# The second projection in two runs of 18 matmuls per quad, and the gate's column sums made by TensorE

## The chip, the cores and the metric

The kernel runs on one core of a Trainium2 chip. The metric is the device time of one execution, in microseconds (us). Five engines work from queues of their own, each in the order in which the program gives it its instructions: TensorE (PE in the profile, its weight loads PEld), VectorE (DVE), ScalarE (ACT), GpSimd (POOL) and SyncE (SP), which only issues transfers here. They wait for each other by semaphores.

## What is computed

Three stages in float32 on 1536 tokens of 512 features: attention in chunks with a few memory rows, then two mixtures of experts that use every expert. The second mixture's gate is normalized eight times in turn over the experts of a token and over all the tokens of an expert.

```python
# mixture 1: E = 4 experts, F = 1024 hidden features
p = domain_probs / (domain_probs.sum(-1, keepdims=True) + 1e-09)
for e in range(E):
    h = np.maximum(x @ w1[e], 0.0)
    out += p[:, e:e + 1] * (h @ w2[e])
...
# mixture 2: E = 8 experts
logits = x @ w_gate
logits = logits - logits.max()
P = np.exp(logits)
for _ in range(8):
    P /= P.sum(1, keepdims=True) + 1e-09
    P /= P.sum(0, keepdims=True) + 1e-09
    P *= N / E
for e in range(E):
    h = np.maximum(x @ w1[e], 0.0)
    out += P[:, e:e + 1] * (h @ w2[e])
```

## The kernel before

**Precision.** Every large product is made of three matmuls on rounded values: an operand is split into hi (a rounded copy, made by ScalarE) and lo (the value less hi, made by VectorE), and `in_three` adds hi x lo, hi x hi and lo x hi.

**Order of the mixtures.** There are four passes (mixture 1 for batch 0 and 1, mixture 2 for batch 0 and 1), of 4, 4, 8 and 8 experts. An expert is four quads, so there are 96 quads, numbered 0 to 95: passes begin at quads 0, 16, 32 and 64. A quad is a 2 x 2 block of the first projection (256 hidden features, 768 tokens), done in seven products instead of eight by Strassen's scheme. Each product is 6 matmuls of 384 columns into the PSUM areas c_ps[0] to c_ps[3]. Two quads fill one buffer h of hidden values, 512 features, called half m.

**The work on a quad.** GpSimd forms four sums of weight blocks (`sum_s`), ScalarE splits the seven stationary blocks (`split_s`, s_hi, L610) and VectorE makes the lo part (s_lo, L749). TensorE runs products 0 to 6. ScalarE copies four partial results out of PSUM (`keep_part`, L628), VectorE adds each to another area (`add`, L768), ScalarE applies the relu and rounds (`hidden`, h_hi, L632), and VectorE makes h_lo (L772). The four (add, hidden) pairs belong to products 2, 5, 6 and 7, counted from one, so the last needs the quad's last product. The first product of the next quad needs its s_lo, and the PSUM areas of the first two pairs.

**The second projection** (`down`) of half m runs during the quads 2m+2 and 2m+3: in each of them three tiles of 128 tokens, each of 4 x 3 matmuls of 512 columns into one of three areas y_ps. It is cut into pieces of three matmuls, and `PIECES` says how many stand behind each product. VectorE adds each finished tile to the result (`accumulate`, L784 to L790). It needs w2 split in the same way (`split_w2`, by ScalarE in L615 and VectorE in L755).

```python
PIECES = (2, 2, 1, 2, 2, 2, 1)
...
                    product(quad, i)
                    for _ in range(PIECES[i]):
                        if m >= 0:
                            down(m, piece // 4, piece % 4)
                        piece += 1
```

**Between passes.** The tokens of the next pass are summed (`sum_t`, `sum_t4` on GpSimd) and split (`split_t`, L623 and L760) in the last quad of a pass (15, 31, 63), each block when the product that last used its buffer is done (`next_tokens`). Behind mixture 1 TensorE transposes the rows (`turn_rows`) and makes the logits, in quads 18 and 33 to 34.

**The gate.** The largest logit over all tokens is found on GpSimd at quad 34 (L368). The eight rounds are cut into nine slots, three in each of quads 35, 36 and 37 (`gates`): VectorE normalizes over experts and sums a token column (`sinkhorn_rows`, L805 to L809), GpSimd sums over the 128 partitions (L372), and VectorE takes the sum up (`sinkhorn_columns`, L813 to L817). GpSimd's wait for a column sum stands in the same queue as `sum_s`.

**The queues.** All orders are written out by hand. w1_raw and w2_raw are single buffers: SP loads w1 of quad q when s_lo of quad q-1 is made, and w2 of half m when the last w2_lo of half m-1 is made.

Of the kernel before, what the change touches and what calls it, by code (L numbers as in the profile page):

```python
# [11 lines left out]
RED = bass.bass_isa.ReduceOp  # L12
# [25 lines left out]
PIECES = (2, 2, 1, 2, 2, 2, 1)  # L38


def build(nc, q, k, v, mem_k, mem_v, domain_probs, a_w1, a_w2, w_gate, b_w1, b_w2, out):
# [37 lines left out]
    with ExitStack() as ctx:  # L79
# [29 lines left out]
        ident = sb("ident", [P, P])  # L109
        gate = sb("gate", [P, TILES, E])  # L110
# [3 lines left out]
        cols = sb("cols", [P, 3 * EB])  # L114
# [24 lines left out]
        csum, ctotal, crec = cols[:, 0:EB], cols[:, EB:2 * EB], cols[:, 2 * EB:3 * EB]  # L139
# [36 lines left out]
        lmax_ready, gmax_ready, nmax_ready, sink_exp = sem("lmax_ready"), sem("gmax_ready"), sem("nmax_ready"), sem("sink_exp")  # L176
        csum_ready, ctotal_ready = sem("csum_ready"), sem("ctotal_ready")
# [5 lines left out]
        for t in range(ST):  # L183
            TURNS[LAST_A[0] + 2, t] = ("turn", 0, t)
        TURNS[LAST_A[0] + 2, 6] = ("logits", 0, 0)
        for t, (dq, i) in enumerate(((1, 0), (1, 1), (1, 2), (1, 4), (2, 0), (2, 1))):
            TURNS[LAST_A[1] + dq, i] = ("turn", 1, t)
        TURNS[LAST_A[1] + 2, 3] = ("logits", 1, 0)
        SINK0 = LAST_A[1] + 3

# [101 lines left out]
        def _(pool):  # L292
# [3 lines left out]
                               pattern=[[-1, P]], channel_multiplier=1).then_inc(ident_ready, 1)  # L296
            pool.memset(k_in[1][:], 0.0).then_inc(k_in_zeroed[1], 1)
# [59 lines left out]
            sum_s(1)  # L357
            for quad in range(ALLQ):
                for p in range(1, PASSES):
                    if quad == QUADS * (FIRST[p] - 1):  # L360
                        sum_t(p)
                    if quad == QUADS * FIRST[p] - 1:
                        sum_t4(p)
                if quad + 2 < ALLQ:
                    sum_s(quad + 2)
                if quad == SINK0 - 1:
                    pool.wait_ge(lmax_ready, 1)
                    pool.partition_all_reduce(gmax, lmax, P, RED.max).then_inc(gmax_ready, 1)  # L368
                if SINK0 <= quad < SINK0 + 3:
                    for it in range(3 * (quad - SINK0), min(3 * (quad - SINK0) + 3, SINKHORN)):  # L370
                        pool.wait_ge(csum_ready, it + 1)
                        pool.partition_all_reduce(ctotal, csum, P, RED.add).then_inc(ctotal_ready, 1)  # L372

        @block.tensor
        def _(pe):
# [91 lines left out]
            def down(m, t, f):  # L467

                y, par = m * ST + t, m % 2
                if t == 0 and f == 0:  # L470
                    pe.wait_ge(h_lo_ready, 8 * (m + 1))
                    pe.wait_ge(w2_lo_ready, 2 * (m + 1))
                if f == 0 and y >= 3:
                    pe.wait_ge(y_taken, y - 2)
                ts = slice(t * P, (t + 1) * P)
                mm = in_three(y_ps[y % 3], h_hi[par][:, f, ts], h_lo[par][:, f, ts], w2_hi[par][:, f, :],
                              w2_lo[par][:, f, :], f == 0, f == 3)
                if f == 3:
                    mm.then_inc(y_summed, 1)

# [47 lines left out]
            for quad in range(ALLQ):  # L528
                m = quad // 2 - 1
                piece = 12 * (quad % 2)  # L530
# [39 lines left out]
        def _(act):  # L570
# [102 lines left out]
            for quad in range(ALLQ):  # L673
                take_turned(quad, 0)
# [4 lines left out]
                take_turned(quad, 1)  # L679
                next_tokens(quad, 1)  # L680
                hidden(quad, 0)
                take_turned(quad, 2)
                keep_part(quad, 1)
                next_tokens(quad, 2)
                take_turned(quad, 3)
                split_w2(quad // 2, quad % 2)
                keep_part(quad, 2)
                next_tokens(quad, 3)
                take_turned(quad, 4)
                keep_part(quad, 3)  # L690
                next_tokens(quad, 4)
                hidden(quad, 1)
                take_turned(quad, 5)
                hidden(quad, 2)
                next_tokens(quad, 5)
                hidden(quad, 3)
                next_tokens(quad, 6)
                if quad == SINK0 - 1:
                    act.wait_ge(nmax_ready, 1)
                    act.activation(sink[:], sink[:], ACT.Exp, bias=nmax).then_inc(sink_exp, 1)  # L700

        @block.vector
        def _(dve):
# [47 lines left out]

            def split_w2(m, j):
                dve.wait_ge(w2_hi_ready, 2 * m + j + 1)
                fs = slice(2 * j, 2 * j + 2)
                dve.tensor_tensor(out=w2_lo[m % 2][:, fs, :], in0=w2_raw[:, fs, :], in1=w2_hi[m % 2][:, fs, :].bitcast(F32),  # L755
                                  op=ALU.subtract).then_inc(w2_lo_ready, 1)
# [54 lines left out]
            def sinkhorn_columns(it):  # L811
                dve.wait_ge(ctotal_ready, it + 1)
                then(dve.tensor_scalar(crec, ctotal, EPS, None, ALU.add))  # L813
                then(dve.reciprocal(crec, crec))
                then(dve.tensor_scalar(crec, crec, N / EB, None, ALU.mult))
# [52 lines left out]
            for quad in range(ALLQ):  # L868
                m, t0 = quad // 2 - 1, 3 * (quad % 2)
                if m >= 1 or quad == 3:  # L870
                    accumulate((quad - 1) // 2 - 1, 3 * ((quad - 1) % 2) + 2)
                if quad == SINK0 + 3:
# [17 lines left out]
                if (quad, 3) in TURNS and TURNS[quad, 3][0] == "logits":  # L890
                    take_logits(TURNS[quad, 3][1])
                gates(quad, 1)
                add(quad, 1)
                hidden(quad, 1)
                if m >= 0:
                    accumulate(m, t0 + 1)
                next_tokens(quad, 4)
                add(quad, 2)
                hidden(quad, 2)
                next_tokens(quad, 5)  # L900
                add(quad, 3)
                hidden(quad, 3)
                next_tokens(quad, 6)
                if (quad, 6) in TURNS:
                    take_logits(TURNS[quad, 6][1])
                if quad == SINK0 - 1:
                    dve.wait_ge(gmax_ready, 1)
                    dve.tensor_scalar(nmax, gmax, -1.0, None, ALU.mult).then_inc(nmax_ready, 1)
                gates(quad, 2)
# [24 lines left out]
```

## Time and profile before

| | |
|---|---|
| median of 3 runs | 1722.59 us (1720.34 to 1725.53) |
| the profiled execution | 1730.89 us |
| its span | 1729.1 us |
| mean granted TensorE clock | 0.963 |
| PE busy | 1626.9 us (94%) |
| DVE busy | 1003.6 us (58%) |
| ACT busy | 690.9 us (40%) |
| POOL busy | 329.8 us (19%) |

The span runs from the first to the last instruction of the program, and the profiled execution's time has 1.8 us around it. Windows and timelines count from the span's start. Matmuls overlap in the profile (one of 384 columns is shown as 0.33 long, and the next starts 0.17 to 0.18 behind it), so starts are to be compared, not lengths. A granted clock (PEclk) of 1.00 is 2.4 GHz, and 0.50 is 1.2 GHz.

### The profile page before, as it was taken

What the parts mean: (1) busy time and instruction counts of PE and PEld (TensorE: products, weight loads), DVE (VectorE), ACT (ScalarE), POOL (GpSimd) and SP (SyncE); (2) the same over time, 40 slices, a digit from 0 to 9 for tenths busy, and PEclk for the clock granted to TensorE, in tenths of its full rate; (3) what the DMA queues carried; (4) which work ended last, traced back from release to release, by engine and by line L of the source; (5) the groups of instructions that cost most, each with busy time, mean ns of one, the idle gap of its engine ahead of it and who ended that gap; (6) DMA issues with size and microseconds to landing.
All of it is one profiled execution on the core that took longest, in us unless ns stands there. A gap on an engine that the chain in (4) does not pass through costs nothing.

```text
span 1729.1 us, 21400 instructions
## 1 busy us (share of the span) xinstructions
PE 1626.9 (94%) x8673; PEld 1448.9 (84%) x8673; DVE 1003.6 (58%) x1445; ACT 690.9 (40%) x1058; POOL 329.8 (19%) x429
## 2 busy tenths in 40 slices
PE   6659999989999989759999999998999999999999
PEld 6648888879888879648888888887888888888887
DVE  5455655664565564536656565657565556556563
ACT  5443344443334443213444434434334443444441
POOL 2211113121111322011111111132111111111110
PEclk9779999999999999889999999999999999999999
DMA  9832122211212221111121222121222121121210
GB/s 161 127 67 85 62 62 72 62 49 49 86 61 62 73 61 49 40 46 49 61 73 62 61 86 62 49 85 49 97 85 61 50 86 61 56 79 62 78 57 37
DMA packets 158930, 117.75 MB, mean 68 GB/s; under 512 B 31336, under 2 KB 129640, under 8 KB 158832
## 3 DMA queue, kind: packets, MB, share of 16 engines
q1 hardware_dynamic: 158832, 116.39, 23.9%
q8 instruction: 68, 1.11, 0.3%
q14 instruction: 30, 0.25, 0.1%
HBM read 113.22 MB, written 3.15 MB: 67 GB/s over the span
## 4 chain that ended last, share of the span: by engine, by line
PE 85%; DVE 5%; SPq 3%; issue 2%; DMA 2%; ACT 1%; POOL 1%; POOLq 0%
PE banks L439 28%; PE banks L441 28%; PE banks L440 28%; SPq L229 1%; DVE t_lo L760 1%; DVE s_lo L749 1%; SPq L228 1%; DMA w_raw<-in_moe_w 1%; PE banks L497 1%; DVE banks L768 1%; ACT h_hi L632 1%; DMA v_bd<-in_mem_v 1%; DVE h_lo L772 1%; PE banks L425 0%; PE banks L489 0%
## 5 line engine op out<-in xcount | busy, mean ns | idle before, releaser
L439 PE MATMUL banks<-t_lo,s_hi 128*128 128x384 f32 x1344 | 459.6, 342 | 35.9 <-DVE h_lo L772 33.3
L439 PE MATMUL banks<-w_lo,h_hi 128*128 128x512 f32 x1152 | 459.7, 399 | 20.6 <-DVE h_lo L772 19.9
L440 PE MATMUL banks<-w_hi,h_hi 128*128 128x512 f32 x1152 | 459.5, 399 | 0.0
L441 PE MATMUL banks<-w_hi,h_lo 128*128 128x512 f32 x1152 | 458.7, 398 | 0.0
L441 PE MATMUL banks<-t_hi,s_lo 128*128 128x384 f32 x1344 | 456.9, 340 | 0.0
L440 PE MATMUL banks<-t_hi,s_hi 128*128 128x384 f32 x1344 | 454.5, 338 | 0.0
L768 DVE TENSOR_TENSOR banks<-banks,part 128x384 f32<-128x384 f32 x384 | 216.3, 563 | 362.7 <-PE banks L441 220.9
L632 ACT ACTIVATE h_hi<-banks 128x384 fp32r<-128x384 f32 x384 | 188.9, 492 | 555.3 <-DVE banks L768 555.3
L628 ACT ACTIVATE part<-banks 128x384 f32<-128x384 f32 x384 | 188.8, 492 | 392.8 <-PE banks L441 392.6
L439 PEld LDWEIGHTS banks<-t_lo,s_hi 128*128 128x128 f32 x1344 | 256.5, 191 | 67.1 <-issue 36.4
L772 DVE SCALAR_TENSOR_TENSOR h_lo<-banks,h_hi 128x384 fp32r<-128x384 f32 x384 | 213.4, 556 | 163.7 <-ACT h_hi L632 163.7
L307 POOL TENSOR_TENSOR w_raw<-w_raw 128x256 f32<-128x256 f32 x96 | 72.3, 753 | 1206.0 <-DMA w_raw<-in_moe_w 1206.0
L440 PEld LDWEIGHTS banks<-t_hi,s_hi 128*128 128x128 f32 x1344 | 256.1, 191 | 28.0
L439 PEld LDWEIGHTS banks<-w_lo,h_hi 128*128 128x128 f32 x1152 | 219.0, 190 | 59.3 <-DVE h_lo L772 35.8
L441 PEld LDWEIGHTS banks<-w_hi,h_lo 128*128 128x128 f32 x1152 | 218.5, 190 | 48.8
L441 PEld LDWEIGHTS banks<-t_hi,s_lo 128*128 128x128 f32 x1344 | 255.8, 190 | 0.0
L790 DVE SCALAR_TENSOR_TENSOR rows<-banks,gate,rows 128x512 f32<-128x512 f32 x258 | 192.3, 745 | 82.1 <-PE banks L441 82.1
L440 PEld LDWEIGHTS banks<-w_hi,h_hi 128*128 128x128 f32 x1152 | 218.8, 190 | 23.2
L749 DVE TENSOR_TENSOR s_lo<-w_raw,s_hi 128x1792 fp32r<-128x1792 f32 x96 | 193.5, 2016 | 0.0
L610 ACT ACTIVATE s_hi<-w_raw 128x1792 fp32r<-128x1792 f32 x96 | 162.6, 1694 | 2.1 <-POOL w_raw L312 2.1
L755 DVE TENSOR_TENSOR w_lo<-w_raw,w_hi 128x1024 fp32r<-128x1024 f32 x96 | 117.0, 1219 | 2.4 <-ACT w_hi L615 2.4
L615 ACT ACTIVATE w_hi<-w_raw 128x1024 fp32r<-128x1024 f32 x96 | 101.0, 1052 | 0.0
(87 smaller groups left out, 642.5 us busy)
## 6 DMA issues: line engine op xcount, KB each, us to landing
w_raw<-in_moe_w SPq DMA_DIRECT2D x192, 256.0 KB, 3.2
w_raw<-in_moe_w SPq DMA_DIRECT2D x48, 1024.0 KB, 7.0
v_bd<-in_v SPq DMA_DIRECT2D x16, 308.0 KB
w_raw<-in_q SPq DMA_DIRECT2D x8, 384.0 KB, 6.0
k_in<-in_k SPq DMA_DIRECT2D x8, 384.0 KB
out_x<-rows SPq DMA_DIRECT2D x12, 256.0 KB, 2.8
v_bd<-in_mem_v SPq DMA_DIRECT2D x16, 48.0 KB
v_bd<-in_v SPq DMA_DIRECT2D x16, 10.0 KB
```

The source lines that it names most:

```text
L439: pe.matmul(out_, lhs_hi, rhs_lo, start=start, stop=False, skip_group_check=chained)
L440: pe.matmul(out_, lhs_hi, rhs_hi, start=False, stop=False, skip_group_check=chained)
L441: return pe.matmul(out_, lhs_lo, rhs_hi, start=False, stop=stop, skip_group_check=chained)
L610: act.activation(s_hi[quad % 2][:], w1_raw[:, 1:PRODUCTS + 1, :, :], ACT.Copy).then_inc(s_hi_ready, 1)
L615: act.activation(w2_hi[m % 2][:, 2 * j:2 * j + 2, :], w2_raw[:, 2 * j:2 * j + 2, :], ACT.Copy).then_inc(w2_hi_ready, 1)
L628: act.activation(part[:, j, :], c_ps[(0, 0, 3, 0)[j]], ACT.Copy).then_inc(part_copied, 1)
L632: act.activation(hidden_at(h_hi, quad, k), c_ps[BLOCKS[k][0]], ACT.Relu).then_inc(h_hi_ready, 1)
L749: dve.tensor_tensor(out=s_lo[quad % 2][:], in0=w1_raw[:, 1:PRODUCTS + 1, :, :], in1=s_hi[quad % 2][:].bitcast(F32), op=ALU.subtract).then_ ...
L755: dve.tensor_tensor(out=w2_lo[m % 2][:, fs, :], in0=w2_raw[:, fs, :], in1=w2_hi[m % 2][:, fs, :].bitcast(F32), op=ALU.subtract).then_inc(w ...
L768: dve.tensor_tensor(out=bank, in0=bank, in1=part[:, (0, 2, 3, 1)[k], :], op=ALU.add).then_inc(c_added, 1)
L772: dve.scalar_tensor_tensor(out=hidden_at(h_lo, quad, k), in0=c_ps[BLOCKS[k][0]], scalar=0.0, in1=hidden_at(h_hi, quad, k).bitcast(F32), op ...
L790: dve.scalar_tensor_tensor(out=dst, in0=got, scalar=by, in1=dst, op0=ALU.mult, op1=ALU.add).then_inc(y_taken, 1)
```

## The change

- The second projection of a quad is no longer spread over all seven products. Its three tiles stand in two runs of 18 matmuls, one behind the fourth product (i == 3) and one behind the seventh.
- ScalarE and VectorE make the split of the next quad's stationary blocks (`split_s`) behind the quad's last `hidden`, where it stood near the quad's beginning. ScalarE's part of `split_w2` follows it, and so do the token splits 2 to 6 of a pass's last quad.
- The lo part of w2 (`split_w2`) moves from VectorE to GpSimd. SP's order of loads is unchanged, and a w2 load now waits for GpSimd's part.
- The gate's sums over the partitions are made by TensorE: a matmul of a matrix of ones with the columns' sums, into PSUM (`column_sums`), read there by VectorE. Two scalings of the reciprocal are folded into one instruction. The sums stand behind the first run, behind the seventh product, and behind the sixth matmul of the second run.
- The largest logit is found with a transpose, a VectorE reduction and a matmul that spreads it (`turn_largest`, `spread_largest`).
- The transposes and logits move by one product, the rescaling of quad 38 moves behind `hidden(quad, 0)`, and `accumulate` moves with the runs.

```diff
-PIECES = (2, 2, 1, 2, 2, 2, 1)
+TILES_BEHIND = 3
...
-        TURNS[LAST_A[0] + 2, 6] = ("logits", 0, 0)
...
+            TURNS[LAST_A[0] + 2, t + 1] = ("turn", 0, t)
+        TURNS[LAST_A[0] + 3, 1] = ("logits", 0, 0)
+        for t in range(ST):
+            TURNS[LAST_A[1] + 1 + t // 3, t % 3 + 1] = ("turn", 1, t)
+        TURNS[LAST_A[1] + 2, 4] = ("logits", 1, 0)
...
+        COLUMN_SUMS = {}
+        for it in range(SINKHORN):
+            COLUMN_SUMS[SINK0 + it // 3, (4, 7, 9)[it % 3]] = it
+        RESCALE = SINK0 + 3
...
+            def split_w2(m, j):
+                pool.wait_ge(w2_hi_ready, 2 * m + j + 1)
+                fs = slice(2 * j, 2 * j + 2)
+                pool.tensor_tensor(out=w2_lo[m % 2][:, fs, :], in0=w2_raw[:, fs, :],
+                                   in1=w2_hi[m % 2][:, fs, :].bitcast(F32), op=ALU.subtract).then_inc(w2_lo_ready, 1)
             for quad in range(ALLQ):
+                if quad + 1 < ALLQ:
+                    sum_s(quad + 1)
...
-                if quad + 2 < ALLQ:
-                    sum_s(quad + 2)
-                if quad == SINK0 - 1:
-                    pool.wait_ge(lmax_ready, 1)
-                    pool.partition_all_reduce(gmax, lmax, P, RED.max).then_inc(gmax_ready, 1)
-                if SINK0 <= quad < SINK0 + 3:
-                    for it in range(3 * (quad - SINK0), min(3 * (quad - SINK0) + 3, SINKHORN)):
-                        pool.wait_ge(csum_ready, it + 1)
-                        pool.partition_all_reduce(ctotal, csum, P, RED.add).then_inc(ctotal_ready, 1)
+                split_w2(quad // 2, quad % 2)
...
+            def turn_largest():
+                pe.wait_ge(lmax_ready, 1)
+                pe.transpose(x_ps[0:1, P:2 * P], lmax, ident[:]).then_inc(lmax_turned, 1)
+
+            def spread_largest():
+                pe.wait_ge(gmax_ready, 1)
+                pe.wait_ge(ones_ready, 1)
+                pe.matmul(x_ps[:, 2 * P:2 * P + 1], ones[0:1, :], gmax[0:1, :], start=True, stop=True).then_inc(gmax_spread, 1)
+
+            def column_sums(it):
+
+                pe.wait_ge(csum_ready, it + 1)
+                if it == 0:
+                    pe.wait_ge(ones_ready, 1)
+                pe.matmul(x_ps[:, 0:EB], ones[:], csum, start=True, stop=True).then_inc(ctotal_ready, 1)
...
+                    if (quad, i) in COLUMN_SUMS:
+                        column_sums(COLUMN_SUMS[quad, i])
                     product(quad, i)
-                    for _ in range(PIECES[i]):
-                        if m >= 0:
-                            down(m, piece // 4, piece % 4)
-                        piece += 1
+                    if i == 3 and m >= 0:
+                        down(m, t0, range(4))
+                        down(m, t0 + 1, range(2))
+                if quad == SINK0 - 1:
+                    turn_largest()
+                if (quad, PRODUCTS) in COLUMN_SUMS:
+                    column_sums(COLUMN_SUMS[quad, PRODUCTS])
+                if m >= 0:
+                    down(m, t0 + 1, range(2, 4))
+                if quad == SINK0 - 1:
+                    spread_largest()
+                if (quad, PRODUCTS + 2) in COLUMN_SUMS:
+                    column_sums(COLUMN_SUMS[quad, PRODUCTS + 2])
+                if m >= 0:
+                    down(m, t0 + 2, range(4))
...
                 keep_part(quad, 0)
                 next_tokens(quad, 0)
+                take_turned(quad, 1)
+                next_tokens(quad, 1)
+                take_turned(quad, 2)
+                hidden(quad, 0)
+                keep_part(quad, 1)
+                take_turned(quad, 3)
+                keep_part(quad, 2)
+                take_turned(quad, 4)
+                keep_part(quad, 3)
+                take_turned(quad, 5)
+                hidden(quad, 1)
+                take_turned(quad, 6)
+                hidden(quad, 2)
+                hidden(quad, 3)
                 if quad + 1 < ALLQ:
                     split_s(quad + 1)
...
                 split_w2(quad // 2, quad % 2)
...
+                for i in range(2, PRODUCTS):
+                    next_tokens(quad, i)
...
+                if quad > 2:
+                    accumulate((quad - 1) // 2 - 1, TILES_BEHIND * ((quad - 1) % 2) + 2)
+                gates(quad, 0)
+                next_tokens(quad, 0)
+                add(quad, 0)
+                next_tokens(quad, 1)
+                hidden(quad, 0)
...
+                gates(quad, 1)
                 if m >= 0:
                     accumulate(m, t0)
...
+                add(quad, 1)
+                add(quad, 2)
+                hidden(quad, 1)
+                add(quad, 3)
+                hidden(quad, 2)
+                hidden(quad, 3)
+                gates(quad, 2)
...
                 if quad + 1 < ALLQ:
                     split_s(quad + 1)
                 next_tokens(quad, 2)
...
                 next_tokens(quad, 3)
...
                 if m >= 0:
                     accumulate(m, t0 + 1)
...
+                for i in range(4, PRODUCTS):
+                    next_tokens(quad, i)
```

## Rows read from the trace of the kernel before

**Rows 1.** Busy time by stretch: window and length, engines (instructions), PEclk, DMA share, GB/s

```profile
152.84:1692.33 1539.49, 1491.54 (x7322) 1328.60 (x7321) 911.69 (x1300) 616.31 (x954) 293.42 (x385) 0.98 0.21 64
957.59:973.26 15.67, 15.67 (x79) 14.10 (x78) 9.44 (x14) 6.47 (x10) 2.87 (x4) 1.00 0.33 101
973.26:989.21 15.95, 15.93 (x80) 14.05 (x78) 9.45 (x14) 6.48 (x10) 2.87 (x4) 1.00 0.11 33
358.21:381.50 23.29, 18.57 (x79) 16.26 (x78) 14.37 (x20) 8.31 (x13) 3.61 (x5) 0.85 0.16 53
381.50:439.75 58.25, 58.25 (x308) 53.09 (x306) 28.60 (x41) 22.78 (x36) 8.59 (x12) 0.94 0.20 64
652.39:694.62 42.23, 42.23 (x227) 38.67 (x226) 19.16 (x28) 16.05 (x26) 6.07 (x9) 0.92 0.17 50
694.62:799.51 104.89, 71.86 (x314) 62.64 (x312) 54.89 (x132) 25.58 (x41) 14.73 (x24) 0.82 0.13 41
```

**Rows 2.** Timeline of quads 49 and 50: start, length, engine, line, what, [idle before]

```profile
971.69 0.33 PE L440 MATMUL banks<-t_hi,s_hi 128*128 128x384 f32 x1
...
972.39 0.34 PE L441 MATMUL banks<-t_hi,s_lo 128*128 128x384 f32 x1
...
972.76 0.57 DVE L768 TENSOR_TENSOR banks<-banks,part 128x384 f32<-128x384 f32 x1 [0.35 <-PE banks L441]
...
973.36 0.49 ACT L632 ACTIVATE h_hi<-banks 128x384 fp32r<-128x384 f32 x1 [1.54 <-DVE banks L768]
...
973.88 0.56 DVE L772 SCALAR_TENSOR_TENSOR h_lo<-banks,h_hi 128x384 fp32r<-128x384 f32 x1 [0.56 <-ACT h_hi L632]
...
974.50 0.50 PE L439 MATMUL banks<-w_lo,h_hi 128*128 128x512 f32 x1
974.51 0.49 ACT L628 ACTIVATE part<-banks 128x384 f32<-128x384 f32 x1 [0.66 <-PE banks L441]
...
974.83 0.39 PE L440 MATMUL banks<-w_hi,h_hi 128*128 128x512 f32 x1
...
974.90 1.70 ACT L610 ACTIVATE s_hi<-w_raw 128x1792 fp32r<-128x1792 f32 x1
...
983.84 0.49 ACT L628 ACTIVATE part<-banks 128x384 f32<-128x384 f32 x1 [1.94 <-PE banks L441]
...
984.43 0.57 DVE L768 TENSOR_TENSOR banks<-banks,part 128x384 f32<-128x384 f32 x1 [1.54 <-ACT part L628]
```

**Rows 3.** Timeline of quad 31, then one line of GpSimd's groups by line

```profile
620.84 2.02 DVE L749 TENSOR_TENSOR s_lo<-w_raw,s_hi 128x1792 fp32r<-128x1792 f32 x1
...
621.00 3.56 POOL L339 TENSOR_TENSOR rows<-rows,t_two 128x768 f32<-128x768 f32 x1 [7.95 <-DVE t_lo L760]
...
622.78 2.60 DVE L760 TENSOR_TENSOR t_lo<-t_two,t_hi 128x768 fp32r<-128x768 f32 x1
...
L331 POOL TENSOR_TENSOR rows<-rows 128x768 f32<-128x768 f32 x4 | 7.4, 1842 | 0.0
```

**Rows 4.** Timeline of quad 35's gate slot, then one line of the DMA issues

```profile
715.51 0.42 POOL L372 PARTITION_ALL_REDUCE cols<-cols  x1 [6.01 <-issue]
715.97 0.17 DVE L813 TENSOR_SCALAR cols<-cols 128x8 f32<-128x8 f32 x1 [12.05 <-POOL cols L372]
...
717.95 0.32 DVE L809 TENSOR_REDUCE cols<-sink 128x8 f32<-128x96 f32 x1
...
w_raw<-in_moe_w SPq DMA_DIRECT2D x192, 256.0 KB, 3.2
```

**Rows 5.** TensorE's gaps in the timeline, and the stretches behind them

```profile
32.66 0.44 PE L425 MATMUL banks<-v_bd,p_t 128*32 128x130 f32 x4 [3.79 <-DMA v_bd<-in_mem_v]
...
1709.23 0.50 PE L439 MATMUL banks<-w_lo,h_hi 128*128 128x512 f32 x1 [1.07 <-DVE h_lo L772]
...
32.10:35.40 3.30, 2.74 (x52) 2.77 (x56) 0.00 (x0) 0.00 (x0) 0.70 (x1) 0.50 1.15 101
1708.20:1728.00 19.80, 16.64 (x72) 13.44 (x72) 5.72 (x8) 0.39 (x1) 0.00 (x0) 1.00 0.20 75
```

More of the change, by code:

```diff
@@ L11 @@
 AX = mybir.AxisListType
-RED = bass.bass_isa.ReduceOp
 CHUNK, LEFT, RIGHT = 32, 16, 8
@@ L109, in build @@
         ident = sb("ident", [P, P])
+        ones = sb("ones", [P, P])
         gate = sb("gate", [P, TILES, E])
@@ L138, in build @@
         tok_sum = small[:, 24:36]
-        csum, ctotal, crec = cols[:, 0:EB], cols[:, EB:2 * EB], cols[:, 2 * EB:3 * EB]
+        csum, crec = cols[:, 0:EB], cols[:, EB:2 * EB]
         lmax, gmax, nmax = small[:, 48:49], small[:, 49:50], small[:, 50:51]
@@ L465, in product, with down @@
                 mm.then_inc(prod_done, 1)
-            def down(m, t, f):
+            def down(m, t, fs):
                 y, par = m * ST + t, m % 2
-                if t == 0 and f == 0:
+                if t == 0 and fs[0] == 0:
                     pe.wait_ge(h_lo_ready, 8 * (m + 1))
                     pe.wait_ge(w2_lo_ready, 2 * (m + 1))
-                if f == 0 and y >= 3:
+                if y >= 3 and fs[0] == 0:
                     pe.wait_ge(y_taken, y - 2)
                 ts = slice(t * P, (t + 1) * P)
-                mm = in_three(y_ps[y % 3], h_hi[par][:, f, ts], h_lo[par][:, f, ts], w2_hi[par][:, f, :],
-                              w2_lo[par][:, f, :], f == 0, f == 3)
-                if f == 3:
+                for f in fs:
+                    mm = in_three(y_ps[y % 3], h_hi[par][:, f, ts], h_lo[par][:, f, ts], w2_hi[par][:, f, :],
+                                  w2_lo[par][:, f, :], f == 0, f == 3)
+                if fs[-1] == 3:
                     mm.then_inc(y_summed, 1)
+            def turn_largest():
[10 more added lines that the diff above has]
+                pe.matmul(x_ps[:, 0:EB], ones[:], csum, start=True, stop=True).then_inc(ctotal_ready, 1)
             def turn_rows(b, t):
@@ L528, in _ @@
             for quad in range(ALLQ):
-                m = quad // 2 - 1
-                piece = 12 * (quad % 2)
+                m, t0 = quad // 2 - 1, TILES_BEHIND * (quad % 2)
                 for i in range(PRODUCTS):
@@ L750, in split_s @@
                                   in1=s_hi[quad % 2][:].bitcast(F32), op=ALU.subtract).then_inc(s_lo_ready, 1)
[L752 to L756, printed above, removed]
             def split_t(p, i):
@@ L812, in sinkhorn_columns @@
                 dve.wait_ge(ctotal_ready, it + 1)
-                then(dve.tensor_scalar(crec, ctotal, EPS, None, ALU.add))
+                then(dve.tensor_scalar(crec, x_ps[:, 0:EB], EPS, EB / N, ALU.add, ALU.mult))
                 then(dve.reciprocal(crec, crec))
-                then(dve.tensor_scalar(crec, crec, N / EB, None, ALU.mult))
                 dst = gate[:, :, EA:E] if it == SINKHORN - 1 else sink[:]
@@ L868, in _ @@
             for quad in range(ALLQ):
[L869 to L872, printed above, removed]
+                m, t0 = quad // 2 - 1, TILES_BEHIND * (quad % 2)
+                if quad > 2:
[5 more added lines that the diff above has]
+                hidden(quad, 0)
+                for i in (1, 4):
+                    if TURNS.get((quad, i), ("",))[0] == "logits":
+                        take_logits(TURNS[quad, i][1])
+                if quad == RESCALE:
                     dve.wait_ge(y_taken, (HALVES * FIRST[2] + 2) * ST)
@@ L877, in _ @@
                     dve.wait_ge(rescaled, ST)
-                gates(quad, 0)
-                next_tokens(quad, 0)
-                add(quad, 0)
+                gates(quad, 1)
                 if m >= 0:
                     accumulate(m, t0)
-                hidden(quad, 0)
-                next_tokens(quad, 1)
+                add(quad, 1)
[5 more added lines that the diff above has]
+                gates(quad, 2)
+                if quad == SINK0 - 1:
+                    dve.wait_ge(lmax_turned, 1)
+                    dve.tensor_reduce(gmax[0:1, :], x_ps[0:1, P:2 * P], AX.X, ALU.max).then_inc(gmax_ready, 1)
                 if quad + 1 < ALLQ:
@@ L887, in _ @@
                 next_tokens(quad, 2)
-                split_w2(quad // 2, quad % 2)
+                if quad == SINK0 - 1:
+                    dve.wait_ge(gmax_spread, 1)
+                    dve.tensor_scalar(nmax, x_ps[:, 2 * P:2 * P + 1], -1.0, None, ALU.mult).then_inc(nmax_ready, 1)
                 next_tokens(quad, 3)
[L890 to L894, printed above, removed]
                 if m >= 0:
                     accumulate(m, t0 + 1)
[L897 to L909, printed above, removed]
+                for i in range(4, PRODUCTS):
+                    next_tokens(quad, i)
             accumulate(ALLM - 2, ST - 1)
```

35 lines of the change are left out of this document (6 added, 29 removed).

## The prediction

> **What bounds the kernel now.** I read the stretches first, cut at the starts of quads (a quad begins with the first matmul of its first product). In quad 49 TensorE is busy for all of 15.67 us, and quad 50 takes 15.95 [rows 1]. Every quad holds the same 42 product matmuls and 36 of the second projection, so 15.67 is the floor that the matmuls alone set. From quad 3 to quad 94 the stretch is 1539.5 us, and 92 floors are 1441.6: the excess is 97.9 us [rows 1]. Its parts, from the same view:
> - Quads that carry nothing special and have an even number lose 0.28 (15.95 against 15.67), and there are 39 of them: 10.9.
> - The first quad behind each change of tokens or mixture (16, 32, 64) takes some 23 us (quad 16 stands for the three), 7.3 to 7.6 over the floor: 22.5 for three.
> - Quads 17 to 19 take 58.25 (11.2 over three floors), 33 and 34 take 42.23 (10.9 over two). They carry the transposes and the logits.
> - Quads 35 to 38, the gate's eight rounds, take 104.9: 42.2 over four floors, with TensorE busy for 71.9.
>
> That makes 97.7. The timeline of quads 49 and 50 then shows the 0.28: h_lo of the quad before ends at 974.44, and the second projection's first matmul starts at 974.50 instead of right behind the product; it takes 0.50 where its neighbour takes 0.39, because its weight load too stood behind the wait [rows 2]. So TensorE is the bound, and a change to its order can gain at most what is in the list; what it can lose has no such limit.
>
> **The change, part by part.** *The second projection behind products four and seven.* The floor stays: the same 78 matmuls. A product costs 6 x 0.175 = 1.05 (four product matmuls start from 971.69 to 972.39, in steps of 0.17 to 0.18 [rows 2]); the other 36 matmuls have 15.67 - 7.35 = 8.32, so 0.231 each, and a run of 18 is 4.16. What goes away is the 0.28 of the even quads: the first of these matmuls now stands three products (3.15 us) later, and h_lo was 0.18 late. Gain 10.9.
>
> *split_s behind the last hidden, on ScalarE and on VectorE.* Today ScalarE makes the next quad's s_hi right behind the first part copy (974.51, then 974.90 [rows 2]), some ten microseconds ahead of its use. Now it comes after hidden(3), which waits for the last add, which waits for the seventh product. The next quad's first product waits for s_lo. So there is a chain from the seventh product to the next first product, and it runs beside 18 matmuls. Count from S, the start of the seventh product's last matmul:
> - S to the last add. A free VectorE starts 0.37 later (972.39, 972.76 [rows 2]). Here it isn't free. From the fifth product's last start: its part is copied after 0.37 and the add starts 0.59 behind the copy's start (983.84, 984.43), so at 0.96; h_hi 0.60 later, h_lo 0.52 later still (972.76, 973.36, 973.88), at 2.08; the engine takes its next instruction 0.08 before one ends (620.84 plus 2.02 against 622.78 [rows 3]), so at 2.56. S is at 2.10. I take 0.46; lower bound 0.37.
> - add to h_hi 0.60, and h_hi to s_hi 0.39 as from 974.51 to 974.90 [rows 2].
> - s_hi 1.70 [rows 2], 0.03 to the next engine (h_hi's end at 973.85, h_lo at 973.88), s_lo 2.02 [rows 3], 0.06 to TensorE (974.44 to 974.50).
>
> Sum 5.26. TensorE is free at 0.17 + 4.16 = 4.33. It waits 0.93, and a start from a wait costs 0.10 more (0.50 against 0.39 [rows 2]): **1.03 per quad**, 94.8 for the 92 quads. Bounds: with 0.37 in the first step, 0.94; above, if one more hand-over of 0.2 is in it (part copy and add stand 0.10 further apart than a copy's 0.49), 1.25. Before, nothing hung on this chain, so the trace has no such wait; it's made of its rows.
>
> *split_w2 from VectorE to GpSimd.* GpSimd takes 1.84 for 768 columns alone [rows 3], so 2.46 for 1024. Its input, w2_hi, comes from ScalarE right behind s_hi; by columns against s_hi (1024 to 1792 in 1.70) that is 1.0, so it is ready while s_lo still runs. At 620.84 VectorE's s_lo began first and took its usual 2.02, GpSimd's instruction came 0.16 later and took 3.56, and VectorE's next two-operand one 2.60 [rows 3]: the second of two stands until the first is through. So s_lo isn't slowed, GpSimd starts at its end and is done 2.5 later; the second projection needs w2_lo 4.3 after the same moment (four products). Hidden with 1.8 to spare; without it, a shortfall would cost once in two quads. VectorE loses 1.2 us of work per quad that was on nobody's path.
>
> The Trainium skill, "GPSIMD Engine Reference", section Key points, says that GpSimd shares its SBUF interfaces with VectorE and contends with instructions that have two SBUF inputs. It does not say who gives way; taken as both being slowed while they overlap, it gives the third rival below, and by it the sum would be some 100 us higher than by the row.
>
> *The loads.* SP's next w1 load waits for s_lo as before. It lands 3.2 after issue [rows 4] and GpSimd's four sums of 256 columns need less than 1 each (1.84 for 768 [rows 3]), so s_summed comes at most 7.2 behind s_lo; ScalarE asks for it 16.7 - 3.8 = 13 behind. The w2 load waits for GpSimd now, 2.5 later than s_lo, and stands ahead only of a w1 load that is due a quad later. Nothing.
>
> *Start, quads 0 and 1.* No second projection exists yet, so nothing covers the chain: quad 1 and quad 2 each begin 5.3 behind S, and after idle of that length the clock is low. In quad 16 idle of 4.7 (23.29 less 18.57 busy) came with a mean clock of 0.85 [rows 1], so 7 us at half, and 7.6 - 4.7 = 2.9 lost: 3.0. Quad 0's products end about 1.2 sooner without split_s between the copies, at S near 118; quad 1 starts at 123.3, its S is at 133.4, quad 2 starts at 138.7 and ends, with 16.7 + 3.0, at 158.4. Before: 152.8. **+5.5.**
>
> *Changes of tokens.* In quads 15, 31 and 63 the splits 2 to 6 of the tokens now stand behind s_lo. The first meets GpSimd's split_w2: ready 2.46 + 0.90 behind s_lo (the 0.90 is 2.60 less the 1.70 behind GpSimd [rows 3]), and its product is due at 2.2. Wait 1.2, restart and a little at the fifth product 0.3: 1.5 each. The old 7.6 came from those splits standing between the adds and the hiddens; they're out of it. 4.5 instead of 22.5.
>
> *Gates.* Today a slot waits for GpSimd's reduction, which had nothing to wait for and yet stood idle 6.01 before 715.51 [rows 4], and s_lo and the sums stand in the same queues. Now TensorE makes the sums. A slot on VectorE is 715.97 to 718.27, 2.30, less one instruction: 2.1. In quads 35 and 36 the third sum is asked for six matmuls (1.4) into the second run, at 13.15 from the quad's start, but its csum comes after hidden(3) and a slot: the second slot can only end at 11.0 (it waits for the sum behind the first run, 8.9), then two adds, hidden(1), the last add at 13.2, hidden(3) at 14.4 to 14.9, slot to 17.0. TensorE waits 3.8; the 12 matmuls left cover s_lo. Such a quad is 20.0, 3.3 over 16.7. Quad 37 has no third sum; s_lo ends at 18.0: 1.3. A gap of 3.79 came before a stretch at 0.50 in the attention part [rows 5], so I add the loss of a stretch at the lower level (1.2 of 2.4 GHz), 3.0, to each of the two: 13.9 in all, against 42.2.
>
> *Transposes and logits* keep their work: 21.6 against 22.1.
>
> **Sum.** New excess 94.8 + 4.5 + 21.6 + 13.9 = 134.8, old 97.9: +36.9, and the start +5.5: +42.4. The profiled execution had 1730.9 (span 1729.1), so 1773.3 for its like; the three runs have a median of 1722.6, so **1765 us**, 2.5% slower. The tail is as before: the split that is gone from VectorE is waited for at GpSimd, 0.8 against 1.07 [rows 5].
>
> **Rivals.**
> - *The chain hides, and the gates' gain is kept* (faster). It needs the wait per quad under (94.8 - 42.4)/92 = 0.57 us, so a chain of 4.8 or less from the seventh product. For it: 42.2 us of gate stall and 22.5 at the token changes are real, and go. Against it: s_hi and s_lo alone are 3.7, and the order written for both queues leaves no way round. With no wait at all: 1765 - 94.8 = 1670. Chance 0.08; another 0.02 for a wait so close to 0.57 that nothing shows.
> - *The clock falls at each wait.* The only gap of this size at speed, 1.07, had the clock at 1.00 for all that followed [rows 5]. If it fell in each quad, 3.0 x 92 = 276: 2040. Chance 0.03.
> - *s_lo is slowed by GpSimd* for the 1.1 us that w2_hi is ready before s_lo ends: 1.1 x 92 = 101, 1866. The three cases like 620.84 speak against it. Chance 0.06.
> - *A further wait inside a quad* of 0.5 us or more, where ScalarE's or VectorE's new order makes a part copy late: over 1800, near 1815. The third product's start has only 0.3 us to spare behind the first part copy. Chance 0.05.
>
> **Numbers.** My forecast has 0.76. Its bounds are 0.94 to 1.25 per quad (1757 to 1785), the clock at the gates (-6) and at the token changes (+9), and a start that may be 5 off. The upper end is 1785 + 9 + 5, so 1800. The lower one is 1757 - 6 - 5 = 1746, and 8 less for a chain whose other hand-overs are 0.09 shorter than I read them: 1738. The other rivals lie outside. A difference under 0.3% can't be told from none here. Faster 0.08, same 0.02, slower 0.90.
>
> **What would show it.** Plain quads of 16.7, even and odd alike, each with one TensorE wait of about 0.9 before its first product, released by VectorE's s_lo. s_lo still 2.02; GpSimd's w2_lo over 3 us, as it stands first. Quads 35 to 38 about 80 us together, with two waits near 3.8 in 35 and 36. Quads 1 and 2 beginning 5.3 behind the product before. I am wrong if the wait before the first product is under 0.57, or if s_lo is longer than 2.1.

## The result and the profile after

The change makes the kernel slower: 1757.35 us (median of 4 runs, 1756.56 to 1760.08) against 1723.44 (4 runs), a ratio of 1.020 with a 95% interval of 1.018 to 1.022. The forecast was 1765, with a range of 1738 to 1800.

Stretches of the kernel after, cut at the starts of quads as in [rows 1] (window and length, busy time of PE, PEld, DVE, ACT, POOL with instructions, granted clock, DMA share, GB/s):

```profile
148.48:1719.73 1571.25, 1485.48 (x7340) 1316.61 (x7340) 811.50 (x1201) 608.11 (x954) 598.82 (x473) 0.99 0.20 63
952.43:969.05 16.62, 15.79 (x78) 13.99 (x78) 8.30 (x13) 6.38 (x10) 6.15 (x6) 1.00 0.11 33
969.05:985.70 16.65, 15.82 (x79) 14.02 (x79) 8.31 (x13) 6.38 (x10) 6.17 (x6) 1.00 0.30 95
364.85:383.59 18.74, 16.32 (x79) 13.89 (x79) 15.77 (x18) 8.59 (x14) 8.19 (x6) 1.00 0.27 85
383.59:446.23 62.64, 60.26 (x307) 54.67 (x307) 25.10 (x38) 22.50 (x36) 18.37 (x16) 0.92 0.14 43
664.58:709.27 44.69, 43.41 (x231) 39.49 (x232) 17.48 (x29) 16.31 (x27) 12.60 (x11) 0.92 0.16 48
709.27:786.06 76.79, 68.17 (x329) 60.06 (x328) 51.71 (x119) 25.34 (x41) 26.66 (x21) 0.96 0.17 55
727.50:730.80 3.30, 3.30 (x9) 2.65 (x9) 1.18 (x3) 0.00 (x0) 2.46 (x1) 0.50 0.51 153
```

The reader is to see four things.
- Plain quads, even and odd, take 16.62 to 16.65. TensorE is busy for 15.8 of it and idle for 0.83. Before, they took 15.67 and 15.95.
- Quad 16, behind a change of tokens, takes 18.74 (23.29 before) and keeps its clock.
- Quads 35 to 38, from 709.27 to 786.06, take 76.8 (104.9 before).
- From quad 3 to quad 94 the sum is 1571.25 (1539.49 before): +31.8.

With +3.8 in quads 0 to 2 (46.4 against 42.6) and -0.5 in the tail, from quad 95's start to the end of the last matmul (33.0 against 33.5), it is +35.0 from the first quad on. That is close to the difference of the medians (+33.9). The two profiled executions differ by 26.9 only, because the attention part, which the change leaves alone, took 110.3 in the one of before and 102.1 in the one of after. Over the traces of all runs of this study it took 100.8 to 110.3, so stretches are compared from the first quad on.

Who waits for whom (total, times, longest), two lines of the waits after:

```profile
PE banks L446 <- DVE s_lo L781: 84.9, 92, 4.9
...
PE banks L503 <- DVE cols L835: 6.3, 2, 3.1
```

The first is the new wait. It came 92 times, and no such line is among the waits of before. The timeline of quad 50's end shows what it hangs on:

```profile
980.43 0.34 PE L448 MATMUL banks<-t_hi,s_lo 128*128 128x384 f32 x1
...
980.61 0.39 PE L446 MATMUL banks<-w_lo,h_hi 128*128 128x512 f32 x1
...
980.91 0.56 DVE L794 TENSOR_TENSOR banks<-banks,part 128x384 f32<-128x384 f32 x1
...
981.50 0.49 ACT L667 ACTIVATE h_hi<-banks 128x384 fp32r<-128x384 f32 x1 [0.63 <-DVE banks L794]
...
981.89 1.69 ACT L645 ACTIVATE s_hi<-w_raw 128x1792 fp32r<-128x1792 f32 x1
...
983.62 2.02 DVE L781 TENSOR_TENSOR s_lo<-w_raw,s_hi 128x1792 fp32r<-128x1792 f32 x1 [1.03 <-ACT s_hi L645]
...
984.48 0.39 PE L448 MATMUL banks<-w_hi,h_lo 128*128 128x512 f32 x1
984.61 3.29 POOL L368 TENSOR_TENSOR w_lo<-w_raw,w_hi 128x1024 fp32r<-128x1024 f32 x1 [8.95 <-ACT w_hi L650]
...
985.70 0.44 PE L446 MATMUL banks<-t_lo,s_hi 128*128 128x384 f32 x1 [0.82 <-DVE s_lo L781]
```

The last matmul of the seventh product starts at 980.43. Then come the last add (980.91), h_hi (981.50), s_hi (981.89) and s_lo (983.62 to 985.64), and the next product starts at 985.70: 5.27 after 980.43, where the prediction added up 5.26. The 18 matmuls between them start from 980.61 to 984.48.

### The profile page after: what moved, and what is told of

Its sections match the earlier page's. It is cut to its first block, busy times and chain, and to the rows that moved or that the text cites. A ratio compares the mean times of both kernels' runs of the same rounds, so it can differ in the third digit from the quotient of the medians.

```text
span 1756.0 us, 21410 instructions
## 1 busy us (share of the span) xinstructions
PE 1617.2 (92%) x8692; PEld 1434.4 (82%) x8692; DVE 898.9 (51%) x1342; ACT 683.0 (39%) x1058; POOL 644.8 (37%) x517
## 3 DMA queue, kind: packets, MB, share of 16 engines
HBM read 113.22 MB, written 3.15 MB: 66 GB/s over the span
## 4 chain that ended last, share of the span: by engine, by line
PE 55%; DVE 20%; ACT 15%; issue 6%; SPq 3%; DMA 1%; DVEq 0%; ACTq 0%
PE banks L446 19%; PE banks L448 17%; PE banks L447 17%; DVE s_lo L781 11%; ACT s_hi L645 9%; DVE banks L794 6%; ACT h_hi L667 3%; ACT part L663 3%; DVE t_lo L786 1%; SPq L236 1%; SPq L235 1%; PE banks L521 1%; DMA v_bd<-in_mem_v 1%; PE banks L513 0%; DVE h_lo L798 0%
## 5 line engine op out<-in xcount | busy, mean ns | idle before, releaser
L368 POOL TENSOR_TENSOR w_lo<-w_raw,w_hi 128x1024 fp32r<-128x1024 f32 x96 | 316.7, 3299 | 858.4 <-ACT w_hi L650 858.4
L446 PE MATMUL banks<-t_lo,s_hi 128*128 128x384 f32 x1344 | 467.5, 348 | 90.7 <-DVE s_lo L781 84.9
L446 PE MATMUL banks<-w_lo,h_hi 128*128 128x512 f32 x1152 | 451.8, 392 | 0.6 <-issue 0.6
L447 PE MATMUL banks<-w_hi,h_hi 128*128 128x512 f32 x1152 | 451.5, 392 | 0.0
L448 PE MATMUL banks<-w_hi,h_lo 128*128 128x512 f32 x1152 | 450.1, 391 | 0.0
L794 DVE TENSOR_TENSOR banks<-banks,part 128x384 f32<-128x384 f32 x384 | 206.8, 561 | 321.8 <-ACT part L663 206.6
L816 DVE SCALAR_TENSOR_TENSOR rows<-banks,gate,rows 128x512 f32<-128x512 f32 x258 | 185.7, 745 | 261.5 <-PE banks L448 261.5
```

The costliest lines, as they stand in the source:

```text
L368: pool.tensor_tensor(out=w2_lo[m % 2][:, fs, :], in0=w2_raw[:, fs, :], in1=w2_hi[m % 2][:, fs, :].bitcast(F32), op=ALU.subtract).then_inc( ...
L446: pe.matmul(out_, lhs_hi, rhs_lo, start=start, stop=False, skip_group_check=chained)
L447: pe.matmul(out_, lhs_hi, rhs_hi, start=False, stop=False, skip_group_check=chained)
L448: return pe.matmul(out_, lhs_lo, rhs_hi, start=False, stop=stop, skip_group_check=chained)
L794: dve.tensor_tensor(out=bank, in0=bank, in1=part[:, (0, 2, 3, 1)[k], :], op=ALU.add).then_inc(c_added, 1)
L816: dve.scalar_tensor_tensor(out=dst, in0=got, scalar=by, in1=dst, op0=ALU.mult, op1=ALU.add).then_inc(y_taken, 1)
```

## The experiments

Each ratio is to runs of the kernel before made beside the run in question. Their median was 1728.34 us for split_early, run12_24, run15_21 and run24_12, and 1724.20 for the others. So times are compared across the two groups, and with the 1757.35 above, by their ratios.

**The split of the next quad put back into the quad (split_early).** One part of the change undone, on both engines:

```diff
                 keep_part(quad, 2)
+                if quad + 1 < ALLQ:
+                    split_s(quad + 1)
...
                 hidden(quad, 3)
-                if quad + 1 < ALLQ:
-                    split_s(quad + 1)
                 split_w2(quad // 2, quad % 2)
...
                 hidden(quad, 0)
+                if quad + 1 < ALLQ:
+                    split_s(quad + 1)
...
-                if quad + 1 < ALLQ:
-                    split_s(quad + 1)
                 next_tokens(quad, 2)
```

> The changed kernel with one part undone: ScalarE and VectorE make the next quad's s_hi and s_lo during the first run of 18 matmuls again (behind the third part copy, and behind hidden 0), and no longer behind the last hidden. Theory of the prediction (the chain from the seventh product through add, h_hi, s_hi and s_lo to the next first product is what costs 0.96 us per quad): the wait before the first product goes, quads take 15.67, and the time falls by 92 x 0.96 = 88 us plus some 4 at the start, to 1665 us, ratio to before 0.967. Rival (the two long runs of 512-column matmuls themselves are slower than the interleaved order, or GpSimd's w2 split slows VectorE): quads stay near 16.6 and the time near 1757. If ScalarE's split waits for GpSimd's sums, which now stand behind its w2 split, there is a new wait inside the quad and quads take 15.9 to 16.3.

1664.32 us, ratio to before 0.963 (0.960 to 0.967). Stretches of its quad 50 and of its quads 35 to 38:

```profile
924.52:940.08 15.56, 15.56 (x80) 14.10 (x79) 8.30 (x12) 6.40 (x10) 5.22 (x6) 1.00 0.31 101
673.02:753.36 80.34, 70.19 (x330) 62.24 (x329) 53.43 (x118) 25.42 (x40) 18.07 (x20) 0.92 0.17 53
```

The wait is gone and the plain quad takes 15.56. So the place of `split_s` alone is what turned a faster kernel into a slower one: 93 us between the medians of this kernel and the changed one, 98 us by the two ratios to the kernel before. The 15.56 is a surprise, 0.11 under what was taken for the floor. GpSimd's weight sums weren't late. In this kernel's timeline s_hi follows the third part copy at once, and GpSimd's w2_lo has no s_lo beside it and takes 2.40:

```profile
922.83 2.40 POOL L368 TENSOR_TENSOR w_lo<-w_raw,w_hi 128x1024 fp32r<-128x1024 f32 x1 [10.26 <-ACT w_hi L650]
...
928.90 0.49 ACT L663 ACTIVATE part<-banks 128x384 f32<-128x384 f32 x1 [0.55 <-PE banks L448]
...
929.29 1.70 ACT L645 ACTIVATE s_hi<-w_raw 128x1792 fp32r<-128x1792 f32 x1
...
931.02 2.02 DVE L781 TENSOR_TENSOR s_lo<-w_raw,s_hi 128x1792 fp32r<-128x1792 f32 x1 [2.51 <-ACT s_hi L645]
```

Quads 35 to 38 take 80.3, 3.5 more than in the changed kernel. The timeline of quad 35 shows where that comes from:

```profile
687.96 2.37 POOL L368 TENSOR_TENSOR w_lo<-w_raw,w_hi 128x1024 fp32r<-128x1024 f32 x1 [12.61 <-ACT w_hi L650]
...
688.46 1.90 DVE L832 TENSOR_SCALAR small<-small 128x12 f32<-128x12 f32 x1
...
691.54 0.60 PE L503 MATMUL banks<-cols,ones 128*128 128x8 f32 x2 [5.08 <-DVE cols L835]
```

A VectorE instruction of the gate's slot, 0.17 long in five of this kernel's eight slots, takes 1.90 here, while GpSimd's w2_lo runs, and ends with it. TensorE then waits 5.08 for the third column sum, where it waits 3.13 in the changed kernel, in which w2_lo begins behind this slot. The same three lines stand in quad 36, so the waits alone make 3.9 of difference. No run moves w2_lo away from the slot in this kernel.

**Runs of 12 and 24 (run12_24), 15 and 21 (run15_21), 24 and 12 (run24_12).** `split_s` stays at the end of the quad; only the cover behind the seventh product is changed.

```diff
+FIRST_RUN = 4    # pieces of three matmuls: 4, 5 or 8
...
                     if i == 3 and m >= 0:
-                        down(m, t0, range(4))
-                        down(m, t0 + 1, range(2))
+                        pieces(m, t0, 0, FIRST_RUN)
...
                 if m >= 0:
-                    down(m, t0 + 1, range(2, 4))
+                    pieces(m, t0, FIRST_RUN, FIRST_RUN + 2)
...
                 if m >= 0:
-                    down(m, t0 + 2, range(4))
+                    pieces(m, t0, FIRST_RUN + 2, 12)
```

> The changed kernel with the runs cut 12 and 24 instead of 18 and 18; nothing else moves. Chain theory: the second run covers 24 x 0.23 + 0.17 = 5.7 of a chain of 5.27, the wait is gone, quads take 15.67, time 1757 - 88 = 1669 us. The gates' third sum now stands 6 matmuls behind as before, so quads 35 and 36 keep a wait near 3.1. Rival (the long runs or their bank order cost the time): quads at 16.6 or more.

> Runs of 15 and 21. Chain theory: three more matmuls of cover take 0.69 from the wait, quads take 16.63 - 0.69 = 15.94, time near 1757 - 63 = 1694 us. Rival (a wait is there or not whatever the cover): 16.6 or 15.67.

> Runs of 24 and 12. Chain theory with the clock kept: six matmuls less of cover add 1.38, quads take 18.0, TensorE's shown gap 0.83 + 1.38 = 2.2, time near 1757 + 127 = 1884 us. Rival (the clock falls once the gap is 2.2 in every quad): quads of 20 and more, granted clock well under 0.9 in plain stretches, time over 2050.

run12_24: 1667.11 us, ratio 0.966 (0.963 to 0.969), and on another occasion (run12_24_again) 1664.57, 0.965 (0.962 to 0.968). Its quad 50 and its quads 35 to 38:

```profile
924.99:940.55 15.56, 15.56 (x80) 14.10 (x78) 8.36 (x13) 6.40 (x10) 6.18 (x6) 1.00 0.32 102
679.34:753.83 74.49, 68.07 (x330) 60.33 (x328) 51.70 (x118) 25.24 (x40) 25.62 (x21) 0.95 0.18 56
```

run15_21, a single run: 1704.38 us, 10 over its expectation. On the same occasion the kernel before was 5 above its median of 1723.44, and a plain quad is 15.97 where 15.94 was expected. Its quad 50:

```profile
945.78:961.75 15.97, 15.82 (x79) 14.02 (x79) 8.30 (x13) 6.39 (x10) 6.15 (x6) 1.00 0.33 99
```

run24_12, a single run: 1954.05 us. Its quads 47 and 48, and the start of the latter in the timeline:

```profile
1011.49:1029.47 17.98, 15.80 (x78) 14.00 (x79) 8.30 (x13) 6.38 (x10) 6.15 (x6) 1.00 0.10 29
1029.47:1049.04 19.57, 17.39 (x79) 15.59 (x79) 8.30 (x13) 6.43 (x10) 6.15 (x6) 0.91 0.26 82
...
1029.47 0.44 PE L447 MATMUL banks<-t_lo,s_hi 128*128 128x384 f32 x1 [2.18 <-DVE s_lo L785]
```

Plain quads by matmuls behind the seventh product: 12: 17.98 where the clock stays; 18: 16.63; 21: 15.97; 24: 15.56. From 12 to 18 that is 1.35 for six matmuls and from 18 to 21 it is 0.66 for three, so 0.22 to 0.23 each, which is the step from one of these matmuls to the next (981.76 is 0.23 behind 981.53 in the timeline of the changed kernel). At 24 the chain of 5.27 is covered. The expectation for 12 and 24, 1884 us, missed by 70 us. Its quads without clock loss are as expected (18.0), and so is the gap (2.18). But every second quad has a mean clock of 0.91, that is about 3.4 us at the lower level, and takes 19.6. So a gap of 2.2 in every quad does cost the clock, as the rival had it, though not each time. What picks the one quad and not the other, the runs don't show.

The second occasion of the 12 and 24 runs, whose figures stand above, was expected thus:

> The runs of 12 and 24 once more, beside the kernel with the moved gate slots on the same chip: 1667 us, quads of 15.56, ratio 0.966.

**The gate's sums alone (gates_alone).** The kernel before, with TensorE's column sums in place of GpSimd's reduction. The edit also folds two scalings of the reciprocal into one instruction, as the change does, and asks for the sums at products of its own:

```diff
+        COLUMN_SUMS = {}
+        for it in range(SINKHORN):
+            slot = it % 3
+            COLUMN_SUMS[SINK0 + it // 3 + slot // 2, (4, 6, 2)[slot]] = it
...
-                if SINK0 <= quad < SINK0 + 3:
-                    for it in range(3 * (quad - SINK0), min(3 * (quad - SINK0) + 3, SINKHORN)):
-                        pool.wait_ge(csum_ready, it + 1)
-                        pool.partition_all_reduce(ctotal, csum, P, RED.add).then_inc(ctotal_ready, 1)
...
+                    if (quad, i) in COLUMN_SUMS:
+                        column_sums(COLUMN_SUMS[quad, i])
                     product(quad, i)
```

> The kernel before with one part of the change: the gate's column sums are made by TensorE (ones times csum), not by GpSimd; the largest logit stays on GpSimd, and so does everything else. The sums stand ahead of products five, seven and, in the next quad, three. Theory: the 42 us that quads 35 to 38 take over four floors come from GpSimd's reduction and its place in the queue of the weight sums, so they shrink to 5 to 12 us: quads 35 to 38 take 68 to 75 instead of 104.9, the time falls by 30 to 37 us to about 1690, ratio 0.980. Rival (the chain of small VectorE instructions sets it): quads 35 to 38 stay over 90.

1686.54 us, ratio 0.978 (0.976 to 0.980). Its quads 35 to 38, and its quad 50:

```profile
690.01:757.29 67.28, 65.35 (x329) 58.48 (x328) 53.36 (x124) 25.47 (x41) 11.48 (x16) 1.00 0.21 63
931.20:947.17 15.97, 15.95 (x79) 14.18 (x78) 9.44 (x14) 6.47 (x10) 2.94 (x5) 1.00 0.11 33
```

Quads 35 to 38 take 67.3 instead of 104.9, with the clock at 1.00, and a plain even quad stays at 15.97: the 37.6 us are the gain of the whole kernel (1686.54 against 1724.20). The sum itself, 0.4 us on GpSimd, was never the price. In the kernel before, two lines in front of those of [rows 4] show what the first sum of quad 35 stood behind:

```profile
697.42 0.36 DVE L809 TENSOR_REDUCE cols<-sink 128x8 f32<-128x96 f32 x1
...
706.55 0.73 POOL L307 TENSOR_TENSOR w_raw<-w_raw 128x256 f32<-128x256 f32 x1 [15.36 <-DMA w_raw<-in_moe_w]
```

csum is done at 697.78. GpSimd waits for the next w1 until 706.55, makes four weight sums, and stands idle for 6.01 before it begins the reduction at 715.51. The run takes away both the place in the queue and the idle time, and doesn't tell their shares apart.

**w2_lo back on VectorE (w2_vector).** The changed kernel with the one edit undone:

```diff
-                split_w2(quad // 2, quad % 2)      # GpSimd
...
                     split_s(quad + 1)              # VectorE
+                split_w2(quad // 2, quad % 2)
                 next_tokens(quad, 2)
```

> The changed kernel with w2_lo back on VectorE, behind s_lo. Theory of the prediction (GpSimd's w2 split stands behind s_lo and is hidden): plain quads stay at 16.63, s_lo at 2.03, time within 5 us of 1757. Where tokens change (quads 16, 32, 64) the first split behind s_lo waits 1.2 for VectorE's own instruction instead of 2.4 for GpSimd's, so the 2.1 us over a plain quad fall to about 1.2: 3 us in all. Rival (GpSimd slows VectorE's instructions and so lengthens the chain): quads shorter by 0.2 or more, time under 1740.

1756.38 us, ratio to before 1.017 (1.014 to 1.020), which can't be told from the changed kernel. Its quad 50 and its quad 16:

```profile
971.87:988.49 16.62, 15.79 (x78) 14.00 (x78) 9.41 (x14) 6.39 (x10) 2.86 (x4) 1.00 0.30 95
371.44:389.09 17.65, 16.19 (x78) 13.87 (x78) 14.68 (x19) 8.59 (x14) 4.77 (x4) 1.00 0.29 90
```

The plain quad is 16.62 either way, so in plain quads GpSimd neither slowed VectorE's s_lo nor was waited for. Quad 16 is 17.65 instead of 18.74, 3.3 us in all three such quads: the first token split behind s_lo really stood behind GpSimd. In the changed kernel's timeline it begins beside w2_lo and takes 3.15, and the next split takes 0.95:

```profile
363.76 3.29 POOL L368 TENSOR_TENSOR w_lo<-w_raw,w_hi 128x1024 fp32r<-128x1024 f32 x1 [6.38 <-ACT w_hi L650]
364.71 3.15 DVE L786 TENSOR_TENSOR t_lo<-t_two,t_hi 128x768 fp32r<-128x768 f32 x1
...
367.79 0.95 DVE L786 TENSOR_TENSOR t_lo<-t_one,t_hi 128x768 fp32r<-128x768 f32 x1
```

**The gate's slots inside the first run (gates_mid).** On top of the runs of 12 and 24:

```diff
-            COLUMN_SUMS[SINK0 + it // 3, (4, 7, 9)[it % 3]] = it
+            COLUMN_SUMS[SINK0 + it // 3, (3, 4, 7)[it % 3]] = it
...
                 if m >= 0:
                     accumulate(m, t0)
+                gates(quad, 2)
                 add(quad, 1)
...
                 hidden(quad, 3)
-                gates(quad, 2)
```

> Runs of 12 and 24 with the gate's slots moved into the first run: sums ahead of product four, ahead of product five and behind the seventh, and the third slot on VectorE ahead of the second add. Expected: the waits near 3.1 in quads 35 and 36 go with the clock loss behind them; a wait of 0.3 for the first sum and up to 1.3 before the next quad stay. Quads 35 to 37 take 48 to 52 us instead of 58.9, time some 8 us under that of the 12 and 24 runs (1659). Rival (the late adds lengthen the chain by the slot's whole 2.1 and more): no gain.

1655.92 us, ratio 0.960 (0.958 to 0.962), beside 0.965 (0.962 to 0.968) for run12_24_again on the same chip. Its quads 35 to 38 and its quad 50:

```profile
674.71:740.50 65.79, 65.04 (x329) 57.91 (x328) 52.07 (x118) 25.43 (x40) 23.87 (x21) 1.00 0.21 63
911.66:927.22 15.56, 15.56 (x79) 14.11 (x78) 8.36 (x13) 6.38 (x10) 6.17 (x6) 1.00 0.34 102
```

65.8 instead of 74.2 to 74.5, and quads 35 to 37 take 50.2, within the expected 48 to 52. It is the fastest kernel of this study, faster than both the one before and the changed one.

## Why the prediction was right, step by step

In the prediction's own terms, excess of quads 3 to 94 over 92 floors of 15.67:

| part | forecast | measured | from |
|---|---|---|---|
| wait before the first product | 94.8 | 88.3 | 92 x (16.63 - 15.67) |
| changes of tokens | 4.5 | 6.3 | 3 x (18.74 - 16.63) |
| transposes and logits | 21.6 | 24.2 | 62.64 + 44.69 - 5 x 16.63 |
| gates | 13.9 | 10.3 | 76.79 - 4 x 16.63 |
| sum | 134.8 | 129.1 | 129.6 by the whole stretch |
| quads 0 to 2, against before | +5.5 | +3.8 | |

- **The chain.** Shown. It took 5.27 as worked out (5.26), each link within 0.02 of its row. Moving the split away (split_early) removes the wait, and a longer cover removes all of it (run12_24) or the 0.66 that three more matmuls cover (run15_21).
- **The floor** was mis-sized. The prediction kept 15.67; the same 78 matmuls take 15.56 when they stand in two runs. So the wait by itself costs 16.63 - 15.56 = 1.07 (forecast 1.03), and the runs give back 0.11 per quad, 10 us in all, which the prediction had at nothing. Together with the 0.28 of the even quads that is 21 us of gain by the new order that was forecast as 11. That the sum came close is in part luck: the wait cost 3.7 us more than forecast (92 x 0.04) and the floor gave back 10.1, and of the terms below the gates and the start were 5.3 too dear and the changes of tokens and the transposes 4.4 too cheap.
- **split_w2 on GpSimd.** As forecast: s_lo took 2.02 with 1.0 us of GpSimd's instruction beside it, and that instruction took 3.29 (2.40 where nothing of VectorE's kind stood beside it, against the 2.46 worked out from 768 columns). The rival in which both are slowed fell with this row and with w2_vector. The cited section, Key points of "GPSIMD Engine Reference" in the Trainium skill, says that the two engines contend in such a case, and the trace agrees. By these rows the one that began first isn't slowed, and the other is.
- **Changes of tokens.** Right in mechanism, 0.6 too small for each (4.5 forecast, 6.3 measured). TensorE's waits in quad 16 after, in the timeline:

```profile
364.85 0.44 PE L446 MATMUL banks<-t_lo,s_hi 128*128 128x384 f32 x1 [0.84 <-DVE s_lo L781]
...
367.92 0.44 PE L446 MATMUL banks<-t_lo,s_hi 128*128 128x384 f32 x1 [0.70 <-DVE t_lo L786]
...
375.29 0.41 PE L446 MATMUL banks<-t_lo,s_hi 128*128 128x384 f32 x1 [0.89 <-ACT part L663]
```

The third product waits 0.7 for the token split, where 1.2 was forecast, and the fifth then waits 0.9 for a part copy, which the prediction had, with the restart, as 0.3.
- **Gates.** Right in mechanism; the wait was 3.13 instead of 3.8, in quad 35 and in quad 36. The sum's instruction, its csum and the s_lo behind it, in the timeline of quad 35 after:

```profile
725.85 0.39 PE L503 MATMUL banks<-cols,ones 128*128 128x8 f32 x2 [3.13 <-DVE cols L835]
...
725.47 0.32 DVE L835 TENSOR_REDUCE cols<-sink 128x8 f32<-128x96 f32 x1
725.72 2.02 DVE L781 TENSOR_TENSOR s_lo<-w_raw,s_hi 128x1792 fp32r<-128x1792 f32 x1
```

csum is done at 725.79, 16.5 into the quad, where the prediction had 17.0. The clock behind it was at 0.50 (1.2 GHz) from 727.50 to 730.80 (last row of the first listing), about half as long as in quad 16 before, from which the prediction took its 3.0. Two waits that are 0.7 shorter and two stretches that cost some 1.6 instead of 3.0 (an estimate: half of 3.3) would make 4.1 less than forecast; measured, it was 3.6 less. gates_alone shows that 37.6 of the old 42.2 us came from GpSimd's reduction with its place in the queue.
- **The start** (quads 0 to 2) took +3.8 instead of +5.5. Quads 1 and 2 begin 5.3 behind the last matmul before them, as forecast (111.17 to 116.43), and the clock is low behind both gaps. But it is low for some 3.4 us and not for 7 (a mean of 0.51 from 116.43 to 119.90, in the stretches of the kernel after). So quads 1 and 2 took 14.06 and 17.99 (forecast 15.4 and 19.7), while quad 0 took 14.35 (forecast 13.0). It is the same term, the loss of 3.0 behind a gap, that was too large at the gates.
- **Transposes and logits** took 2.6 more than forecast. The clock was low there for longer than before (a mean of 0.92 over 62.6 us, against 0.94 over 58.3 [rows 1]); what lengthened it was not tried.
- **The rivals.** The shortest of the 92 waits was 0.73, so none came under 0.57, and the faster one fell. The clock held at waits of 0.83 in every plain quad. A further wait inside plain quads didn't come: split_early and run12_24 run at the floor, where it would show.

## What to carry to other kernels

A preparation that is put behind the last step of an iteration becomes part of the chain from this iteration's last product to the next one's first. Add up that chain, hand-overs included, and compare it with the work that stands beside it, before the order is changed; here 5.27 stood against 4.3, and 0.23 us of cover per matmul could be moved there for nothing. A change made of several edits deserves a run of each. In this one, the place of `split_s` took 98 us. Against it, quads 35 to 38 gave back 28 in the changed kernel (38 when the gate's sums were moved alone), and, read from the stretches and not from runs of their own, the order in two runs gave 21 and the changes of tokens 16.

## What the runs showed that was not expected

- The same 78 matmuls take 15.56 us in two runs and 15.67 in seven groups. The step between two 512-column matmuls is 0.228 in the long runs and 0.231 in groups of three and six (means of the differences of starts over quads 40 to 59 of run12_24 and of the kernel before, second projection to second projection). That isn't the rule, though. In gates_alone, which keeps the seven groups, quads without the 0.28 take 15.67 again, but with 0.228 between two 512-column matmuls and 0.177 between two of 384, where the kernel before and run12_24 both have 0.175. What the runs show is the length of the quad; what sets it is open.
- Waits of 0.83 us in every quad left the clock at 1.00. Gaps of 2.18 in every quad took it down in every second one, for about 3.4 us each.
- GpSimd's two-operand instruction and VectorE's s_lo exclude each other in the order in which they begin: s_lo 2.02 with or without it when it is first, GpSimd's 2.40 alone and 3.29 behind it. In split_early s_lo was second three times, in quads 12, 28 and 60 (at 295.33, 0.85 before GpSimd's instruction of 294.33 ended), and took 2.73. VectorE's instruction L832 on twelve columns, with one input, took 1.90 instead of 0.17 behind w2_lo.
